# Phase 1 of a three-stage attention and MoE kernel: queries by feature block and turned on VectorE, sums in halves of the array, another order of the first batch

## What is computed

```python
q_s = softmax(q, over the 64 features of a head)
k_s = softmax(k, over the 576 tokens)
x = q_s @ (k_s.T @ v)                                # per head, heads side by side: 512 features
xn = (x - mean) / sqrt(var + 1e-6) * g_ln            # per token
x = x + relu(xn @ w_ch1) @ w_ch2                     # 512 -> 2048 -> 512
out = sum over the top 2 of 4 experts of gate * (causal attention_e(x) @ wo_e)
```

## Time and profile before

| What | us |
|---|---|
| Runs, median (lowest to highest of 3) | 1414.82 (1414.41 to 1416.0) |
| The profiled execution | 1413.79 |
| Its span | 1411.7 |
| Start, until the first product of the first chunk | 54.2 |
| First chunk, until its successor's residual | 180.9 |
| Phase 1 ends, phase 2 begins | about 975 |

### The profile page before, as it was taken

One profiled execution on the slowest core, in us unless ns is written; L12 is line 12 of the kernel. 1 busy time (PEld: TensorE's weight loads), 2 busy tenths in 40 slices (PEclk: granted clock), 3 DMA queues, 4 the chain that ended last, 5 costly groups with the idle time before them and its releaser, 6 DMA issues.

```text
span 1411.7 us, 19604 instructions
## 1 busy us (share of the span) xinstructions
PE 1336.7 (95%) x7392; PEld 1157.6 (82%) x7392; DVE 664.8 (47%) x1628; ACT 498.4 (35%) x1092; POOL 229.6 (16%) x260
## 2 busy tenths in 40 slices
PE   4789999999999999999999999998789999999996
PEld 3568788888888888888888888887789999999984
DVE  5557444344344344344244222113577767767662
ACT  2323322222222122122122111122356667666663
POOL 0111000000000000000000000021455535543331
PEclk9799999999999999999999999999899999999997
DMA  7271130240230330320510100302212012010001
GB/s 156 66 152 67 41 94 1 60 75 1 72 64 1 75 61 8 89 38 1 110 25 8 60 0 0 105 1 49 68 35 68 16 53 68 32 37 35 34 31 38
DMA packets 147018, 70.48 MB, mean 50 GB/s; under 512 B 126704, under 2 KB 130800, under 8 KB 146928
## 3 DMA queue, kind: packets, MB, share of 16 engines
q1 hardware_dynamic: 146928, 69.23, 20.2%
HBM read 49.29 MB, written 19.92 MB: 49 GB/s over the span
## 4 chain that ended last, share of the span: by engine, by line
PE 88%; DVE 5%; issue 3%; ACT 2%; POOL 1%; SPq 1%; DMA 1%; POOLq 0%; DVEq 0%; ACTq 0%
PE hb L1165 27%; PE yb L1264 27%; PE sc L1165 18%; PE ob L1376 3%; PE tb L1358 3%; PE pa L1165 3%; PE pa L1200 2%; PE pa L1228 1%; PE pa L1214 1%; DVE w_lo L870 1%; PE yb L1252 1%; DMA ksb<-in_k_dram 1%; SPq L401 1%; POOL prob L627 1%; PE pa L1178 1%
## 5 line engine op out<-in xcount | busy, mean ns | idle before, releaser
L981 DVE SCALAR_TENSOR_TENSOR hid_lo<-hb,hid_hi 128x512 fp32r<-128x512 f32 x144 | 99.5, 691 | 459.4 <-ACT hid_hi L704 459.0
L704 ACT ACTIVATE hid_hi<-hb 128x512 fp32r<-128x512 f32 x144 | 86.0, 597 | 552.7 <-PE hb L1165 552.7
L1264 PE MATMUL yb<-hid_hi,w_hi 128*128 128x512 f32 x576 | 233.4, 405 | 0.0
L1165 PE MATMUL hb<-xn_hi,w_hi 128*128 128x512 f32 x576 | 229.5, 398 | 1.4 <-issue 1.4
L1165 PE MATMUL hb<-xn_hi,w_lo 128*128 128x512 f32 x576 | 225.7, 392 | 0.0
L1165 PE MATMUL hb<-xn_lo,w_hi 128*128 128x512 f32 x576 | 225.6, 392 | 0.0
L1264 PE MATMUL yb<-hid_hi,w_lo 128*128 128x512 f32 x576 | 225.5, 392 | 0.0
L1264 PE MATMUL yb<-hid_lo,w_hi 128*128 128x512 f32 x576 | 225.3, 391 | 0.0
L1165 PEld LDWEIGHTS hb<-xn_hi,w_hi 128*128 128x128 f32 x576 | 109.1, 189 | 23.4 <-issue 1.8
L1165 PEld LDWEIGHTS hb<-xn_hi,w_lo 128*128 128x128 f32 x576 | 108.9, 189 | 23.5
L1264 PEld LDWEIGHTS yb<-hid_hi,w_lo 128*128 128x128 f32 x576 | 108.5, 188 | 23.6
(11 more groups left out here) (154 smaller groups left out, 2371.2 us busy)
## 6 DMA issues: line engine op xcount, KB each, us to landing
y_scratch<-ysb SPq DMA_DIRECT2D x36, 256.0 KB, 2.1
ksb<-in_k_dram SPq DMA_DIRECT2D x32, 256.0 KB, 4.5
qsb<-in_q_dram SPq DMA_DIRECT2D x32, 256.0 KB, 5.2
vsb<-in_v_dram SPq DMA_DIRECT2D x32, 256.0 KB, 4.4
stage<-in_moe_w_ch_dram SPq DMA_DIRECT2D x16, 512.0 KB, 4.4
out_dram<-osb SPq DMA_DIRECT2D x32, 256.0 KB, 2.0
y_in<-y_scratch SPq DMA_DIRECT2D x28, 288.0 KB, 3.8
ksb<-in_k_dram SPq DMA_DIRECT2D x8, 128.0 KB, 4.3
```

What stands on the lines that cost most here:

```text
L704: act.activation(HID[f % 2][0][:], hb[f % 2][:], ACT.Relu).then_inc(sems["hhi_a"], 1)
L981: dve.scalar_tensor_tensor(out=lo[:], in0=hb[f % 2][:], scalar=0.0, in1=plain(hi[:]), op0=ALU.max, op1=ALU.subtract).then_inc(sems["hlo_v" ...
L1165: ins = pe.matmul(dst, l, r, start=(n == 0), stop=(n == len(terms) - 1))
L1264: ins = pe.matmul(yb[j][:], l, r, start=False, stop=(f == FT - 1 and m == 2), skip_group_check=True)
```

## The change

- The queries are loaded by four DMAs into `qx`, with 32 tokens and 32 features to a block: partition = token within a group of 32, for each of four (half of the heads, half of the features). Each run in DRAM is now 32 numbers, 128 bytes. All 576 tokens of a batch are loaded, for even batches too.
- The maxima are taken over 32 features at a time, exchanged between neighbouring groups of partitions (four small copies) and combined.
- Behind the exponential DVE turns every 32 by 32 block (`qT`, four instructions on 128 by 576), which puts the features on the partitions. PE's transposes of the queries, ACT's copies and `qsum` go.
- `key_sums`: each head's product has 64 weight columns and 65 streamed ones (values and a column of ones), alternately into the lower and the upper half of the output partitions.
- `token_sums`: each head's product uses 64 of the array's rows, alternately the lower and the upper ones, with 128 tokens as weight columns and 65 streamed columns; the 65th, a column of ones in `KV`, gives the queries' sum. Every batch has five tiles now, the fifth of 64 new tokens; its tail is stored to `x_tail` for every batch (`store_tail`).
- `ln`, `xn` and the `T` steps stand one half step earlier.
- The first batch: keys 3 and 4 and the values are issued by ACT; `qmax` stands ahead of `ksub` on DVE; sums and turns have banks of their own (`FIRST_KV`, `FIRST_X`, `FIRST_T`); ACT takes the first two weight pieces behind the exponentials, DVE piece 0 between variance and inverse deviation; POOL waits for `xn`; the keys of batch (0, 1) are issued before pieces 6 and 7.

```diff
         ksb = sb("ksb", [P, NT, D], F32, st1)
-        qsb = sb("qsb", [P, NT, D], F32, st1)
-        qeT = [sb(f"qeT{n}", [P, HP, P], F32, st1) for n in range(2)]
-        kmx = sb("kmx", [P, D], F32, st1)
-        kvbd = [sb(f"kvbd{n}", [P, HP, P], F32, st1) for n in range(2)]
+
+
+
+        NG = S // 32
+        qx = sb("qx", [P, HP, NG, 32], F32, st1)
+        with ExitStack() as st:
+            kmx = sb("kmx", [P, D], F32, st)
+        xsb = sb("xsb", [P, CT, D], F32, st1)
...
-        q_v = q.rearrange("(p x) h s d -> x p s h d", x=2)
+        q_v = q.rearrange("(p x) (y g) (n r) (z c) -> x p y z r g n c", x=2, y=2, r=32, z=2)
...
+        FIRST_KV, FIRST_X, FIRST_T = yb[0], [YB[:, 2:4, :], HB, PA, YB[:, 0:2, :], PA], [yb[2], yb[3], hb[0], hb[1]]
+        KVW = HP * (HD + 1)
...
-        ORDER = ["kmx0", "kmx1", "kmaxT", "kbc", "ksub0", "ksub1", "qmax", "qsub0", "qsub1", "kv", "kvn", "qsum",
-                 "X0", "X1", "X2", "X3", "X4", "X5", "ln", "xn", "T0", "T1", "T2", "T3"]
+        ORDER = ["kmx0", "kmx1", "kmaxT", "kbc", "ksub0", "ksub1", "qmax", "qsub0", "qsub1", "kv", "kvn", "qT",
+                 "X0", "X1", "X2", "X3", "X4", "ln", "xn", "T0", "T1", "T2", "T3"]
         HALF = dict(zip(ORDER, (3, 4, 6, 8, 9, 10, 11, 12, 13, 14, 15, 16,
-                                17, 18, 19, 20, 21, 22, 23, 24, 25, 26, 27, 28)))
+                                17, 18, 19, 20, 21, 22, 23, 24, 25, 26, 27)))
...
+            def load_k(st, tiles=range(NT)):
+                for t in tiles:
...
             def load_q(st):
-                for t in range(CT):
-                    sp_.dma_start(qsb[:, t, :].rearrange("p (h d) -> p h d", h=H), q_v[st[1], st[0], tok(t)]).then_inc(q_in, 16)
-                if st[1]:
-
-                    sp_.wait_ge(xt_out, st[0] * 16 + 16)
-                    for x in range(2):
-                        sp_.dma_start(qsb[x * TAIL : (x + 1) * TAIL, CT, :].rearrange("p (h d) -> p h d", h=H),
-                                      q_v[x, st[0], CW:S]).then_inc(q_in, 16)
+                for b in range(4):
+                    sp_.dma_start(qx[b * 32 : (b + 1) * 32], q_v[st[1], st[0], b // 2, b % 2]).then_inc(q_in, 16)
 
             def load_piece(n):
                 for m in uses_before(n)[-1:]:
...
@@ -451,9 +457,7 @@
                     if first:
                         for n in range(10, NPC):
                             load_piece(n)
-                    if st[1]:
-                        need(sp_, "x_v", st, 5)
-                        sp_.dma_start(xt_dram[st[0]], qsb[:, CT, :]).then_inc(xt_out, 16)
+                    store_tail(st)
                     if not is_last(following(st)):
                         need(sp_, "xn_t", st, CT)
                         load_k(following(st))
...
-            load_k((0, 0))
+            load_k((0, 0), range(3))
             load_q((0, 0))
-            load_v((0, 0))
             sp_.dma_start(gsb[:], g_ln.rearrange("(k p) -> p k", p=P), allow_slow_non_contiguous=True).then_inc(g_in, 16)
-            for n in range(EARLY):
+            for n in range(EARLY - 2):
                 load_piece(n)
             need(sp_, "xn_t", (0, 0), CT)
             load_k((0, 1))
+            store_tail((0, 0))
+            for n in range(EARLY - 2, EARLY):
+                load_piece(n)
...
-            need(pool, "ones_g", (0, 0), 2)
+            need(pool, "ones_g", (0, 0), 1)
+            need(pool, "xn_v", (0, 0), CT)
             for n in range(1, EARLY, 2):
                 low_piece(n)
...
-            for s in ORDER[: ORDER.index("X5")] + ORDER[ORDER.index("ln") :]:
-                step(s, (0, 0))
-                if s == "X0":
-                    high_piece(0)
-                if s == "X1":
-                    high_piece(1)
+
+            START = (0, 0)
+            for t in range(3, NT):
+                act.dma_start(ksb[0 : ROWS[t], t, :].rearrange("p (h d) -> p h d", h=H), k_v[0, 0, tok(t)]).then_inc(k_in, 16)
+            for t in range(NT):
+                act.dma_start(VS[0][0 : ROWS[t], t, :, 0:HD], v_v[0, 0, tok(t)]).then_inc(v_in, 16)
+            for s in ("ksub0", "ksub1", "qsub0", "qsub1"):
+                step(s, START)
+            high_piece(0)
+            high_piece(1)
+            step("ln", START)
+            for t in range(CT):
+                need(act, "xn_t", START, t + 1)
+                act.copy(XN[0][0][:, :, t * P : (t + 1) * P], FIRST_T[t][:].rearrange("p (g c) -> p g c", g=KT)).then_inc(sems["xnhi_a"], 1)
...
+            def normalize_kv(st, sums):
+                need(dve, "kv_mm", st, 1)
+                kv = sums[:, 0:KVW].rearrange("p (g c) -> p g c", g=HP)
+                dve.tensor_scalar(krs[:].rearrange("p (g o) -> p g o", o=1), kv[:, :, HD : HD + 1], EPS_SUM, None, ALU.add).then_inc(sems["krs_v"], 1)
+                need(dve, "krs_v", st, 1)
+                dve.reciprocal(krs[:], krs[:]).then_inc(sems["krs_v"], 1)
+                need(dve, "krs_v", st, 2)
+                dve.tensor_tensor(KV[st[1]][:, :, 0:HD], kv[:, :, 0:HD], krs[:].rearrange("p (g o) -> p g o", o=1).to_broadcast([P, HP, HD]), ALU.mult).then_inc(sems["kv_v"], 1)
...
+            def tokens(st, t, sums):
+
+                r = slice(P - ROWS[t], P)
+                need(dve, "x_mm", st, t + 1)
+                both = sums[r, :, 0:KVW].rearrange("p x (g c) -> p x g c", g=HP)
...
+                dve.tensor_scalar(xrs[r].rearrange("p x (g o) -> p x g o", o=1), both[:, :, :, HD : HD + 1], EPS_SUM, None, ALU.add).then_inc(sems["xrs_v"], 1)
+                need(dve, "xrs_v", st, 2 * t + 1)
+                dve.reciprocal(xrs[r], xrs[r]).then_inc(sems["xrs_v"], 1)
+                need(dve, "xrs_v", st, 2 * t + 2)
+                to = xsb[:, t, :] if t < CT else ksb[r, CT, :]
+                if t == CT:
+
+                    dve.wait_ge(xt_out, st[0] * 32 + (st[1] * 16 + 16))
+                dve.tensor_tensor(to.rearrange("p (x g d) -> p x g d", g=HP, x=2), both[:, :, :, 0:HD],
+                                  xrs[r].rearrange("p x (g o) -> p x g o", o=1).to_broadcast([ROWS[t], 2, HP, HD]), ALU.mult).then_inc(sems["x_v"], 1)
+                if t < CT:
+                    need(dve, "x_v", st, t + 1)
+                    token_stats(st, t)
+                else:
+                    dve.sem_inc(sems["bst_v"], 1)
...
                 if s == "qmax":
-                    dve.wait_ge(q_in, st[0] * (16 * (2 * CT + 2)) + (16 * CT if st[1] == 0 else 16 * (2 * CT + 2)))
-                    for t0, t1 in groups(st):
-                        dve.tensor_reduce(stat(qmx, t0, t1), per_head(qsb, t0, t1), AX.X, ALU.max).then_inc(sems["qmx_v"], 1)
+                    dve.wait_ge(q_in, st[0] * (8 * 16) + (st[1] * 64 + 64))
+                    for n in range(2):
+                        dve.tensor_reduce(qmx[:, 2 * n * NG : (2 * n + 2) * NG], qx[:, 2 * n : 2 * n + 2].rearrange("p g n c -> p (g n) c"), AX.X, ALU.max).then_inc(sems["qmx_v"], 1)
+                    need(dve, "qmx_v", st, 2)
+
+                    other = xsb[:, 0, 0 : HP * NG]
+                    need(dve, "x_t", st, 0)
+                    need(dve, "kmax_b", st, 1)
+                    for b in range(4):
+                        dve.tensor_copy(other[32 * b : 32 * b + 32], qmx[32 * (b ^ 1) : 32 * (b ^ 1) + 32]).then_inc(sems["qmx_v"], 1)
+                    need(dve, "qmx_v", st, 6)
+                    dve.tensor_tensor(qmx[:], qmx[:], other, ALU.max).then_inc(sems["qmx_v"], 1)
                 if s in ("qsub0", "qsub1"):
-                    need(dve, "qmx_v", st, 2 + st[1])
-                    for t in ((0, 1), range(2, queries(st)))[int(s[4])]:
-                        dve.tensor_tensor(per_head(qsb, t, t + 1), per_head(qsb, t, t + 1), spread(qmx, t, t + 1), ALU.subtract).then_inc(sems["qsub_v"], 1)
+                    need(dve, "qmx_v", st, 7)
+                    for g in ((0, 1), (2, 3))[int(s[4])]:
+                        dve.tensor_tensor(qx[:, g], qx[:, g], qmx[:, g * NG : (g + 1) * NG].rearrange("p (n o) -> p n o", o=1).to_broadcast([P, NG, 32]), ALU.subtract).then_inc(sems["qsub_v"], 1)
                 if s == "kvn":
...
+                    normalize_kv(st, pa[0])
+                if s == "qT":
+                    for g in range(HP):
+                        need(dve, "qexp_a", st, g + 1)
+                        dve.transpose(q_part(g), q_part(g)).then_inc(sems["qT_v"], 1)
+                if s[0] == "X":
+                    tokens(st, int(s[1]), PA)
...
-            for s in ORDER[: ORDER.index("X5")] + ORDER[ORDER.index("ln") :]:
-                step(s, (0, 0))
-                if s == "X1":
-                    low_piece(0)
+            START = (0, 0)
+            for s in ("kmx0", "kmx1", "kmaxT", "qmax", "ksub0", "ksub1", "qsub0", "qsub1"):
+                step(s, START)
+            normalize_kv(START, FIRST_KV)
+            step("qT", START)
+            for t in range(CT):
+                tokens(START, t, FIRST_X[t])
+            variance(START)
```

(106 more changed lines are left out.)

154 lines of the change are left out of this document (62 added, 92 removed).

## The result

The changed kernel takes **1421.51 us** (median, 1418.01 to 1423.25) beside 1414.63 (1412.87 to 1416.0) of the kernel before, a ratio of 1.0045, 95% interval 1.0034 to 1.0056: 7 us slower. The prediction said 1402.8 and faster. The time lies in its range, the direction is wrong. The profiled execution took 1420.8, its span 1419.0.

What follows compares the result with a forecast made beforehand. PE bounds the steady part, a chain of waits the start, and the first chunk has holes. Gains of 3.7 (steady), 0.7 (start) and 7.6 (first chunk) make 12.0 off 1413.79, median 1402.8 us; own range 1395 to 1413, overall 1388 to 1424.

Steps and rivals of the forecast that it cites:

- The work on PE: Steady batches: key sums 2.65 and five token tiles of 1.24 each, saving PE 1.15 us (even) and 2.9 (odd).
- rival 1: Token sums: row halves load weights one after the other, 0.87 more a tile, 30.5 us more, 1433; chance 0.10.
- Rival 2: Key sums: records cannot start closer than 0.0545 us on average, 14.6 us more, 1417.4; chance 0.10.
- The turn and its wait: Steady batches: four query turns on DVE at 0.75 each make PE wait 1.4 us before the first token sum.
- Rival 3: DVE turns run at half rate, 1.35 each, 19 us more, 1422; chance 0.10.
- Steady, together: Three even and three odd batches: PE's savings less a wait of 1.4 each, 3.7 us gained.
- The start: Before the first long product: queries land at 21.5, chain of 32 behind them, 0.7 us gained, range -2 to +4.
- The first chunk: First chunk: earlier keys and the odd batch's saving, less new waits on DVE, gain 7.6 us, range 2 to 11.
- The 9.2: First chunk: issuing the next batch's keys before pieces 6 and 7 frees the 6.89 hole and 2.3 of slow clock.
- ln and xn one half step earlier are hidden: Steady batches: DVE waits 4.48 us before this hidden layer, so the earlier steps cost nothing; some tenths if cover fails.
- Rivals 4 and 5: 4: token weights hidden, 14.4 us less, 1388, chance 0.10. 5: queries land early at 15, 6.5 less, 1396, chance 0.10.

Runs made afterwards that it cites:

- e10: Changed kernel with query turns two half steps earlier, ln, xn and token turns one half step later, and 960 unused bytes: 1396.73 us.
- e9: Changed kernel with 960 unused bytes ahead of the values' buffer of even batches and nothing else: 1412.52 us.
- e1_pad: Changed kernel with 32 unused bytes a partition ahead of the second xn buffer and the weights, nothing else: 1421.42 us.
- e4_before_pad: Kernel before the change with 32 unused bytes added and not one instruction changed: 1419.85 us, ratio 1.0041.
- e8: Changed kernel with query turns two half steps earlier, 992 unused bytes, keys of (0, 1) again behind pieces 6 and 7: 1413.25 us, 7.0 more than without that reordering.
- e7: Changed kernel with query turns two half steps earlier, 992 unused bytes, and ln, xn and token turns one half step later: 1403.78 us.
- e15: e10 with DVE's weight pieces of the first chunk behind the steps of their block instead of ahead: 1386.82 us, ratio 0.9803.
- e12: e10 with 192 unused bytes instead of 960: 1396.75 us.

## Why the prediction was wrong, by its own steps

**The work on PE: right in kind, 0.4 us a batch short.** The key sums' 80 records took 2.63 and lengthened the next block by 0.22 (2.94): 2.85 against 2.65. A token tile took 1.04 and lengthened the next block by 0.26 (2.98): 1.30 against 1.24. So the row halves do run side by side, and rival 1 (2.1 a tile) fell. Rival 2 fell too: the key sums' records start 33 ns apart (2.63/80), below the 54 ns of the earlier trace rows. The 62 ns per matmul that the Trainium skill, page "TensorE: Matmul & The Clock Gate", section "Wait — 56ns, not 53.3ns?", gives with hardware decode off did not bind here, as the 33 ns show; the ≈25 ns that the section gives as the least distance agree with them. With stall and placement taken away (e10: 101.43 and 101.39) an even batch saves 0.74 and an odd one 2.47, where 1.15 and 2.9 were said. Over six batches that is 9.6 instead of 12.2.

**The turn and its wait: right.** A turn took 0.736 (predicted 0.75), the hole was 1.34 to 1.36, and hole and late block together cost 1.44 (102.86 in e9 without a clock drop, 101.41 in e10), where 1.4 was said. Rival 3 (1.35 a turn) fell.

**The clock behind that wait: missed.** The prediction priced the hole by its length. In three of six batches the clock fell to 1.2 GHz for 3.4 us right behind it, and the block took 4.54 instead of 2.98: 1.6 each (1.58 by e9's even chunks), more than the hole. The earlier trace rows had shown the same thing behind the old hole (a block of 4.37), and the prediction used it there as a gain, but did not ask it of the holes that the change adds. Whether it falls behind one hole of 1.35 differs from batch to batch and run to run (none of the odd chunks' in e9, all three in the changed kernel and in e1_pad); what decides it is open.

**The placement: missed, and by no view of before to be seen.** The change freed memory, `W1` moved by 960 bytes, and the odd chunks' first layer runs 3% slower: in (3, 1) 1.23, in the other three 1.0 each. The even chunks, whose last 24 products of the first layer read `XN[1]` too, lose 0.2 each (103.06 against 102.86 in e9): 4.8 us together, and e4_before_pad lost 5.4. e4_before_pad has the placement without the change, e9_after_960 the change without the placement.

**Steady, together.** Work -9.6, stall 6 x 1.44 = +8.6, placement 3 x 1.0 + 3 x 0.2 + 1.23 = +4.8, clock 3 x 1.6 = +4.8: +8.6, and the table's lines give 3 x 3.23 - 3 x 0.80 + 1.23 = +8.5. Predicted was -3.7. So of the 12.2 between the two, placement and clock, which the prediction put at nothing, make 9.6, and the work that was put too low 2.6.

**The start: right.** The queries landed at 20.05 (predicted 21.5) and the chain behind them took 31.9 (predicted 32):

```profile
20.05 2.61 DVE L953 TENSOR_REDUCE qmx<-qx 128x36 f32<-128x1152 f32 x2 [3.43 <-DMA qx<-in_q_dram]
...
43.54 1.67 DVE L861 SCALAR_TENSOR_TENSOR w_lo<-stage,gsb,w_hi 128x256 fp32r<-128x256 f32 x4
```

The 1.67 answers to the 3.73 of the earlier trace rows, as predicted.

**The first chunk: the term that failed most.** Predicted -7.6, measured +1.05, 8.65 apart. The 9.2 were about right (e8: 7.0 by the medians, where 9.2 - 1.2 = 8.0 was said). What failed is the list of what is late next. Holes were put at 1.2 (key broadcast), 2.8 (first token sum), 3.2 (third: 0.5 more than the 2.7 of before) and the old 1.0 (tokens' turn), 8.2 in all; they measured 1.57, 3.61, 3.21 and 3.90, 12.3. Most of the miss is the last: "ln and xn one half step earlier are hidden" was read off a steady batch, and in the first chunk DVE's weight piece of 3.80 at 141.41 stands right ahead of the variance. e7 shows it: one half step later, 3.90 become 1.65. The rest is the clock again: at half for 13.6 us (110.4, 127.4, 147.9), before for 10.2 (79.3, 130.5). Each of the three begins inside or up to 2 us behind a hole of over 3 us. Taking e15's first chunk less its holes as the bare work, 104.35 - 2.7 = 101.7, the changed kernel's 119.85 leaves 119.85 - 101.7 - 12.3 = 5.9 for 13.6 us at half. The same sum for before, with 103.86 as bare work and 10.6 of holes, leaves 4.3 for 10.2: about the same 0.43 us per us. Two traces of one schedule agree: e10 and e12 have the same 9.5 us of holes in the first chunk, the clock at half for 10.2 and 6.8, and take 115.75 and 114.20. The prediction had taken 2.3 of the 4.3 away and added nothing for the new holes; 5.9 - 2.0 = 3.9, with the holes' 4.1 and the work's 0.4, makes 8.4 of the 8.65.

**Rivals 4 and 5** did not come either (a token tile at 1.30 and not 0.83, queries at 20.05 and not 15). None of the rivals named the clock or the placement. The slower side was put on the array and on DVE's rate (rivals 1 to 3), while the trace had the clock's price in a row of its own.

## What to carry to other kernels

A hole of PE is to be priced with the block behind it: in this kernel 1.35 us of waiting brought 1.6 more on half of its occurrences, and moving one step two places earlier on the engine that was waited for gave all of it back (14 us). An order that is harmless in the steady loop must be stepped through again in the one chunk that carries extra work on the same engine: putting that work behind the step that others wait for was worth 10 us. And when a change alters buffer sizes, compare the pace of products that it does not touch; if it moved, look at the distance between operand and weights before looking anywhere else.

## What the runs showed of the hardware

- The first layer's products of 512 columns start 226.6 ns apart where streamed operand and weights lie a multiple of 256, 512 or 2048 bytes apart, and mostly 231 to 235 ns at odd multiples of 32 and of 64; at an odd multiple of 128 they alternate between 229 and 237. An odd multiple of 32 was tried for both buffers of tokens, the others for `XN[1]`.
- The granted clock fell to half for 3.4 us behind a hole of 1.35 us in a stretch in which PE was otherwise always busy, in some batches and not in others; at the first chunk's holes of 3 us and more for 3.4 to 6.8. One drop of 3.4 us cost 1.58.
- A weight piece on DVE, with two operands in SBUF, took 1.67 alone and 3.81 while POOL worked on its own for 2.54. The Trainium skill, page "GPSIMD Engine Reference", section "1. Specifications", names such a contention for DVE instructions with two SBUF inputs; the two rows agree with it.
- Four turns of 128 by 576 on DVE took 2.75 together and 0.736 each; the next began before the one ahead had ended.
